# Attention and gated layer on one core: softmax normalised after the product with the values, and nested loops replaced by one straight schedule of slots

## The reference, cut to what matters

```python
# attention: B, H, S, D = 4, 8, 576, 64
scores = scale * np.matmul(q, k.transpose(0, 1, 3, 2))
cum = np.cumsum(np.maximum(s, 0.0), axis=-1)
bias = -(cum[:, :, :, None] - cum[:, :, None, :])
scores = np.where(causal, -1e9, scores + np.minimum(bias, 0.0))
attn = np.exp(scores - scores.max(axis=-1, keepdims=True))
attn = attn / (attn.sum(axis=-1, keepdims=True) + 1e-09)
x = np.matmul(attn, v)                       # heads put side by side: 576 x 512
# gated layer, x_prev is x shifted by one token
k = np.maximum((mu_k * x + (1 - mu_k) * x_prev) @ w_k, 0.0)      # 512 -> 1024
v = k * k @ w_v                                                  # 1024 -> 512
r = 1.0 / (1.0 + np.exp(-((mu_r * x + (1 - mu_r) * x_prev) @ w_r)))
x = r * v
# mixer
u = x + (np.maximum(x.transpose(0, 2, 1) @ w_tok1, 0.0) @ w_tok2).transpose(0, 2, 1)
out = u + np.maximum(u @ w_ch1, 0.0) @ w_ch2
```

## Time and profile before

| | us |
|---|---|
| median of 3 runs | 1021.73 |
| lowest and highest | 1020.29, 1023.51 |
| profiled execution, its span | 1019.8 |
| two turns of attention alone (5.84 to 133.10) | 127.3 |
| six turns of attention beside gated steps (133.10 to 557.80) | 424.7 |
| the last two gated steps and the mixer | 462.0 |
| PE, DVE, ACT, POOL busy over the span | 915.7, 610.7, 387.0, 379.8 |

### The profile page before, as it was taken

How to read it: one execution, slowest core, us unless ns; L and a number is a source line. 1 busy time by engine, 2 the same in 40 slices (tenths; PEclk the granted TensorE clock), 3 DMA queues, 4 the chain that set the end, 5 groups by cost and what they waited for, 6 DMA issues and landing times.

```text
span 1019.8 us, 21589 instructions
## 1 busy us (share of the span) xinstructions
PE 915.7 (90%) x6645; PEld 843.9 (83%) x6645; DVE 610.7 (60%) x1532; ACT 387.0 (38%) x1048; POOL 379.8 (37%) x713
## 2 busy tenths in 40 slices
PE   6777689888889988898888999899999999999997
PEld 4565578777878877787778998899999999999997
DVE  4878867978788788779787764422333142313222
ACT  3555545455455365464563443221112111211110
POOL 4643466576575665655674651800000000000000
PEclk9978779999999899999999999999999999999999
DMA  7412021121121121220201313210001001000000
GB/s 264 123 36 67 17 60 48 31 75 46 46 58 41 41 58 41 66 55 29 64 0 55 128 36 108 87 47 25 1 23 54 15 23 46 23 0 24 1 24 24
DMA packets 79948, 51.19 MB, mean 50 GB/s; under 512 B 60320, under 2 KB 69088, under 8 KB 79904
## 3 DMA queue, kind: packets, MB, share of 16 engines
q1 hardware_dynamic: 79904, 50.63, 16.8%
HBM read 41.10 MB, written 9.51 MB: 50 GB/s over the span
## 4 chain that ended last, share of the span: by engine, by line
PE 60%; DVE 18%; issue 11%; ACT 5%; POOL 3%; DVEq 1%; DMA 1%; SPq 1%; POOLq 0%; ACTq 0%
PE psum L137 48%; PE psum L686 5%; DVE z L1071 3%; ACT z L871 3%; DVE z L1086 3%; PE psum L669 3%; DVE p_t L1094 2%; PE psum L656 2%; DVE z_sum L1080 2%; DVE x_mix L1131 1%; PE psum L789 1%; DVE x_all L1104 1%; PE psum L769 1%; POOL xm_lo L558 1%; DVE z_inv L1082 1%
## 5 line engine op out<-in xcount | busy, mean ns | idle before, releaser
L871 ACT ACTIVATE z<-z,z_min 128x128 f32<-128x128 f32 (+4 forms) x160 | 95.6, 598 | 124.2 <-DVE z_min L1071 124.2
L1230 DVE SCALAR_TENSOR_TENSOR hid_lo<-psum,hid_hi 128x288 fp32r<-128x288 f32 x96 | 43.9, 457 | 131.7 <-ACT hid_hi L989 131.7
L137 PE MATMUL psum<-u_hi,c_hi 128*128 128x288 f32 x384 | 116.1, 302 | 2.9 <-DVE u_lo L1220 2.9
L669 PE MATMUL psum<-ident,z 128*128 128x128 f32 (+2 forms) x480 | 67.1, 276 | 54.5 <-DVE p_t L1094 41.7
L137 PE MATMUL psum<-hid_hi,c_hi 128*128 128x288 f32 x384 | 113.9, 297 | 0.0
L137 PE MATMUL psum<-hid_hi,c_lo 128*128 128x288 f32 x384 | 113.3, 295 | 0.0
L137 PE MATMUL psum<-hid_lo,c_hi 128*128 128x288 f32 x384 | 113.1, 295 | 0.0
L137 PE MATMUL psum<-u_hi,c_lo 128*128 128x288 f32 x384 | 113.1, 295 | 0.0
L137 PE MATMUL psum<-u_lo,c_hi 128*128 128x288 f32 x384 | 113.0, 294 | 0.0
L669 PEld LDWEIGHTS psum<-ident,z 128*128 128x128 f32 (+2 forms) x480 | 48.9, 147 | 76.3 <-issue 76.1
L521 POOL TENSOR_SCALAR z<-cum_k,cum_qp 128x128 f32<-128x128 f32 (+4 forms) x160 | 95.1, 603 | 42.1 <-PE psum L669 22.7
(11 more groups left out here) (114 smaller groups left out, 2462.3 us busy)
## 6 DMA issues: line engine op xcount, KB each, us to landing
cum_k<-cum_scratch SPq DMA_DIRECT2D x32, 288.0 KB, 3.4
q_raw<-in_q SPq DMA_DIRECT2D x32, 144.0 KB, 2.4
k_raw<-in_k SPq DMA_DIRECT2D x32, 144.0 KB, 2.6
mixed_scratch<-gate SPq DMA_DIRECT2D x32, 144.0 KB, 1.8
x_t<-mixed_scratch SPq DMA_DIRECT2D x8, 576.0 KB, 4.4
out<-o_sb SPq DMA_DIRECT2D x24, 192.0 KB, 2.1
v_raw<-in_v SPq DMA_DIRECT2D x32, 128.0 KB, 2.3
c_raw<-in_moe_w_ch SPq DMA_DIRECT2D x4, 768.0 KB, 6.5
```

Of the source, the lines that this page charges most:

```text
L137: done = nc.tensor.matmul(out, w[a][0:r, tw, w_cols], x[b][0:r, tx, x_cols], start=first and n == 0 and m == 0, stop=last and n == len(til ...
L669: done = nc.tensor.transpose(t_bank[h][0:rows(kb), kb * r:(kb + 1) * r], z_view(h, i, kb * P, rows(kb)), ident[0:r, 0:r])
L871: nc.scalar.activation(w, w, ACT.Exp, bias=z_min[0:r, h, i:i + 1], scale=-1.0, accum_out=z_sum[0:r, i, h:h + 1]).then_inc(exp_done[h], 1)
L1230: nc.vector.scalar_tensor_tensor(hid[1][:, f % 3, :], s_bank[f % 2][:, 0:HALF], 0.0, hid[0][:, f % 3, :].bitcast(F32), ALU.max, ALU.subtra ...
```

## The change

It has three parts.

1. **Normalising.** `normalise` goes. The weights are transposed as the exponential left them. DVE computes the reciprocals of the sums per part (`invert`, two small instructions for three or two blocks), POOL copies each reciprocal 64 times side by side (`spread`, into `inv_rep`), PE transposes that into a `t_bank` (`inverses_t`, uses `nA` for part 0 in bank 0 and `nB` for part 1 in bank 1), and `outputs` multiplies the finished `x_all` by it, with one DVE instruction that frees the bank.
2. **Fewer, wider instructions.** One ACT and one DVE instruction splits what one bank holds, often of both heads (`HOLDS`); the first two query blocks are scored in one piece; POOL masks both heads at once; the key block of 64 is padded with zeros (`p_last`).
3. **The schedule.** `TURN` and the loops go. Slots are counted from 0 to 198; `PAIR_AT` says in which slot a pair begins, and the tables `PE_AT`, `ACT_AT`, `DVE_AT`, `POOL_AT` say in which slot after that each engine does which piece. The first four pairs begin every 7 slots and so overlap by four; the gated layer begins in slot 31 instead of 42. After that a turn still has 21 slots and two pairs: one, here called A, begins in slot 18 of the turn before, and the other, B, in slot 7. All waits are for constants. The mixing for a step stands in slots 10 to 20 of the turn before it; two of its eight parts used to stand at the start of the step's own turn. The order in a slot is still: attention, gated layer, mixing.

```diff
-TURN = [[("q", 0, 0)], [("k", 0, 0)], [("s", 0, 0)], [("s", 0, 1)],
...
+GATE_AT = 31
+PERIOD = 7
+PAIR_AT = [PERIOD * p if p < 4 else GATE_AT - 3 + (p - 4) // 2 * TURN_SLOTS + p % 2 * 10 for p in range(PAIRS)]
...
+PE_AT = {0: ["q"], 1: ["k"], 2: ["s1"], 3: ["s2"], 4: ["s3"], 5: ["s4", "w1"], 6: ["s5", "w2"], 7: ["nA", "vA"],
+         8: ["w3"], 9: ["w4"], 10: ["nB", "vB"]}
+ACT_AT = {0: ["q"], 1: ["k"], 2: ["e1"], 3: ["e2"], 4: ["e3"], 5: ["w1"], 6: ["w2", "e5"],
+          8: ["oA", "w3"], 9: ["w4"], 11: ["oB"]}
+DVE_AT = {0: ["q"], 1: ["k"], 2: ["s1"], 3: ["s2"], 4: ["s3"], 5: ["s4", "w1"], 6: ["s5", "w2", "rA"],
+          8: ["oA", "w3"], 9: ["w4", "rB"], 11: ["oB"]}
...
+PE_RANK, ACT_RANK, DVE_RANK, POOL_RANK = "sqkwnv", "oqkwe", "osqkwr", "xbv"
...
+T_USES = {"q": [("q0", 0), ("q1", 1)], "k": [("k0", 0), ("k1", 1)], "w1": [("w0", 0), ("w1", 1)],
+          "w2": [("w2a", 0), ("w2b", 1)], "nA": [("nA", 0)], "w3": [("w3a", 1), ("w3b", 0)],
+          "w4": [("w4a", 1), ("w4b", 0)], "nB": [("nB", 1)]}
...
+            def spread(p, part):
...
+                nc.gpsimd.tensor_copy(inv_rep[:, 0:b - a, :, :],
+                                      z_inv[:, a:b, :].unsqueeze(3).to_broadcast([P, b - a, 2, D])).then_inc(inv_spread, 1)
...
+            def bank_free(p, name):
+
+                if T_NTH[p, name] > 1:
+                    pe.wait_ge(t_free[T_BANK[name]], T_NTH[p, name] - 1)
...
+            def inverses_t(p, part):
+                name = "nA" if part == 0 else "nB"
+                pe.wait_ge(inv_spread, p * 2 + part + 1)
+                bank_free(p, name)
...
-            def normalise(p, i):
...
-                    w = z_view(h, i, 0, n)
-                    nc.vector.tensor_scalar(w, w, z_inv[0:r, i, h:h + 1], None, ALU.mult).then_inc(p_ready[h], 1)
...
+            def outputs(p, part):
...
+                x = x_all[:, x_part(p, part)]
+                nc.vector.tensor_tensor(x, x, t_bank[bank][:, 0:PART_W[part]], ALU.mult).then_inc(t_free[bank], 1)
...
-            with act.Fori(2, STEPS) as j:
-                for u, slot in enumerate(TURN):
-                    for piece, x, i in slot:
-                        attend(j, x, piece, i)
-                    last_mixes(j - 2, u)
-                    gated_turn(j - 2, u, True)
+            for slot in range(TWO_LEFT):
+                attend(slot)
+                if slot in SPLIT_SLOTS:
+                    weight_hi(SPLIT_SLOTS.index(slot))
+                if slot >= GATE_AT:
+                    step, u = divmod(slot - GATE_AT, TURN_SLOTS)
+                    gated(step, u)
+                    mixes(step + 1, u, MIX_IN_TURN)
+                mixes(0, slot, FIRST_MIX)
```

More of the change, by code:

```diff
@@ L36 @@
 EPS = 1e-9
-QA, QB = 3 * P, S - 3 * P
+AT = [min(i * P, S) for i in range(NBLK + 1)]
+SIZE = [AT[i + 1] - AT[i] for i in range(NBLK)]
+Z_AT = [sum(AT[1:i + 1]) for i in range(NBLK + 1)]
+Z_COLS = Z_AT[NBLK]
+PARTS = [(0, 3), (3, NBLK)]
+PART_AT = [AT[a] for a, _ in PARTS]
+PART_W = [AT[b] - AT[a] for a, b in PARTS]
 GROUPS = CT + FT + CT
@@ L77 @@
 LAST_RECIPROCALS = {3 + n: 1 for n in range(2 * CT)}
-MIX = VALUE
 POOL_LO = 3
[L80 to L90, removed]
+GATE_AT = 31
+PERIOD = 7
+PAIR_AT = [PERIOD * p if p < 4 else GATE_AT - 3 + (p - 4) // 2 * TURN_SLOTS + p % 2 * 10 for p in range(PAIRS)]
+LAST_SLOT = GATE_AT + STEPS * TURN_SLOTS
+TWO_LEFT = GATE_AT + (STEPS - 2) * TURN_SLOTS
+FIRST_MIX = [10, 11, 17, 18, 24, 25, 30, 31]
@@ new lines, with count_t_uses @@
+T_BANK = {name: bank for uses in T_USES.values() for name, bank in uses}
+HOLDS = {"w0": (0, (0, 1), 0, 1), "w1": (1, (0, 1), 0, 2), "w2a": (2, (0,), 0, 3), "w2b": (2, (1,), 0, 3),
+         "w3a": (3, (0,), 0, 4), "w3b": (3, (1,), 0, 4), "w4a": (4, (0, 1), 0, 4), "w4b": (4, (0, 1), 4, 5)}
+def count_t_uses():
+    nth, nth_split, seen, split = {}, {}, [0, 0], [0, 0]
+    for slot in range(LAST_SLOT):
+        for p, piece in pieces(PE_AT, PE_RANK, slot):
+            for name, bank in T_USES.get(piece, []):
+                seen[bank] += 1
+                nth[p, name] = seen[bank]
+                if name[0] != "n":
+                    split[bank] += 1
+                    nth_split[p, name] = split[bank]
+    return nth, nth_split, seen
@@ new lines, in weights_t @@
+            def weights_t(p, name):
+                bank = T_BANK[name]
+                i, heads, first, end = HOLDS[name]
+                for h in heads:
+                    pe.wait_ge(exp_done[h], p * NBLK + i + 1)
+                bank_free(p, name)
+                pe.sem_inc(passed["pe"], 1)
+                r = SIZE[i]
+                for n, (h, k) in enumerate((h, k) for h in heads for k in range(first, end)):
+                    keys = z_view(h, i)[:, AT[k]:AT[k + 1]]
+                    done = nc.tensor.transpose(t_bank[bank][0:SIZE[k], n * r:(n + 1) * r], keys, ident[0:r, 0:r])
+                done.then_inc(t_filled[bank], 1)
@@ new lines, in values @@
+            def values(p, part):
+                q_end = PART_AT[part] + PART_W[part]
+                for h in range(2):
+                    if part == 0 and h == 0:
+                        pe.wait_ge(v_split, p + 1)
+                    for name in (("w2a", "w2b"), ("w4a", "w4b"))[part]:
+                        pe.wait_ge(t_free[T_BANK[name]], T_NTH[p, name])
+                    if p or part:
+                        pe.wait_ge(o_added[h], p * 2 + part)
+                    blocks = [b for b in range(NBLK) if AT[b] < q_end]
+                    for b in blocks:
+                        q0 = max(PART_AT[part], AT[b]) - PART_AT[part]
@@ L1183, in last_mixes, with mixes @@
[L1183 to L1193 removed]
+            def mixes(step, slot, at):
+                for m in range(2 * CT):
+                    if at[m] == slot:
+                        mix(step, m)
```

705 lines of the change are left out of this document (337 added, 368 removed), and 5 rows, old and new, of the table TURN.

## The result

The changed kernel takes 1072.02 us (median of 4 runs, 1066.31 to 1078.32), the kernel before in the same session 1022.62: 1.048 times as long, with a 95% interval of 1.0434 to 1.0527. The forecast was 1035, with a range to 1054. The direction was right and the size was not.

A forecast was written before the change was run, and what follows sets the result against it. It took a turn to be bound by PE's own work plus bank hand-overs among PE, ACT and DVE. 1019.8 - 12 + 27 - 2 = 1033 for the span, 1035 for the median; 8-in-10 range 992 to 1054.

The forecast's parts named there:

- part one: Up to the start of the gated layer: gate begins at 121 and not 133.1, -12 us.
- six turns: Turns of attention beside gated steps: more PE idle time and added transposes, +4.5 us a turn, +27 us.
- the rest: After the six turns: step 7's mixing no longer waits at the turn's start, -2 us; otherwise the same.
- median over the profiled span: The median of the runs lies 1.9 us over the profiled span.
- The waits found in the orders: PE's idle time in a turn, read from the order of each engine: 13.1 us against 9.0.
- the period of 27: Part one, slot 10 to slot 31: three periods of 7 slots, one pair each, taken as 27 us each.
- comes and goes: Low clock in part one, given 2 us in the sum for the gate's start.
- The wait for the mixing: Step 7, at the turn's start: the mixing is no longer waited for, -2 us.
- DVE's relief: DVE's busy time: loses some 97 us, and must fall by 90 to 105 in any case.
- The port and the clock: Rival: POOL holds up small DVE instructions, or low clock in each turn, +8 us a turn; 1059 us, chance 0.09.
- The waits go: Rival: waits go with the normalising, new ones mostly covered; -16 us in the turns, -16 in part one; 988, chance 0.27.
- what DVE does as a sum decides nothing by itself: In a turn: the limit is PE's own work plus moments when PE, ACT and DVE hand a bank around.

The follow-up runs named there:

- e10: Changed kernel with 7, 4 and 7 transposes for nobody ahead of three waits of PE in a turn; 1038.1 us.
- e6: Kernel before the change with its normalising product cut to one column, weights left unnormalised; 977.5 us.
- e2: Changed kernel with 14, 8 and 14 transposes for nobody ahead of three waits of PE in a turn; 1035.5 us.
- e11: Kernel before the change with one more DVE instruction a pair, ahead of the normalising, to lengthen a wait of PE; 1043.7 us.
- e7: Changed kernel with 12 instead of 4 transposes for nobody at the end of each slot of part one; 1060.6 us.
- e3: Changed kernel without its normalising: no reciprocals, copies, transposes or products of them, outputs left unnormalised; 950.5 us.
- e9: Changed kernel's order and wider instructions with the old normalising of the weights on DVE ahead of the transposes; 1020.2 us.
- e5: Changed kernel with ACT's copy of the output's lo half one slot earlier and PE's values ahead of the reciprocals' transposes; 983.7 us.
- e1: Changed kernel with only ACT's copy of the output's lo half one slot earlier, ahead of that slot's gated reads; 1036.1 us.
- e12: Changed kernel with 14 transposes for nobody ahead of the third weights' second half alone; 1066.2 us.

## Why the prediction was wrong, step by step

| term | forecast | measured |
|---|---|---|
| part one | -12 | +2.8 |
| six turns | +27 | +38.7 |
| the rest | -2 | +3.1 |
| median over the profiled span | 1.9 | 7.6 |

The last line is no term of the kernel: the profiled execution, at 1066.3, was the shortest of the four runs. The four differences, 14.8, 11.7, 5.1 and 5.7, make up the 37 us between 1035 and 1072.

- **The waits found in the orders: right.** 13.1 us of idle time a turn were listed, and 10.8 were measured; 4.5 was taken as net with the transposes. At the full clock a turn grew from 68.4 to 72.0 (e10), by 3.6, or 21.5 in six turns. The orders of four engines, with durations from the trace, gave each of the five large waits to 0.6 us; of the small ones about half came (0.45 for 0.9, 0.50 for 1.0). One small slip: at 1.07 us for eight, five transposes are 0.67 us and not 0.55, 0.2 more a turn.
- **The step that failed is the clock, which the sum took as unchanged.** "Such a reading counts some waits that swallow one another, so I take +4.5", with the low clock only at the end of the range and in a rival at 0.09. Measured: the six turns stood 28.9 us over six times 71.97, where before it was 11.6 over six times 68.39. The 17 between them are the clock; with the 21.5 that is the 38.7. This split is an estimate: in e6, at the full clock, every second turn of the old order takes 1.3 more (64.6 for 63.3), and with that the clock's part is 21 and the rest 18. The hint was there: the list held two waits of 2.4, longer than any in the earlier trace rows, and the prediction itself set a turn at 0.93 beside one at 1.00. e2 and e10 show that filling the waits gives the clock back, and e11 that longer ones cost it in the old kernel.
- **Part one: 15 us off.** The gate began at 136.8, outside the 108 to 134 given for it; the same code began it between 133.6 and 140.3, so some 3 of the 15 can be chance. Slot 10 began at 42.5 and not at 38, as pair 0's values and the keys' bank come in between: 4.5. From there to the gate it took 94.3 and not 83. In e7, at a clock of 0.97, the same stretch took 85.4, so 9 of the 11 are the clock again, as far as two single profiles show, and the period of 27 was nearly right (28.5). That the low clock "comes and goes" for 2 us was the mis-sized term.
- **The rest: 5 us off.** The wait for the mixing, 1.7 us, went as forecast. But PE waited 1.49 us for a read of the gate in step 6, and 2.02 for a `k_lo` on DVE where it had been 0.46. No run tries this; that they come from what else DVE and ACT do at those places is argued.
- **DVE's relief: 72 and not 97 us**, outside the 90 to 105 given "in any case". The new instructions cost as forecast (product 0.543 and 0.35, POOL's copy 0.6) or less (the small ones 11.0 us in all for 16), each form for itself:

```profile
L571 POOL COPY inv_rep<-z_inv 128x384 f32<-128x384 f32 x16 | 8.8, 551 | 49.1 <-DVE z_inv L1109 49.1
```

```profile
L1129 DVE TENSOR_TENSOR x_all<-x_all,psum 128x384 f32<-128x384 f32 x16 | 8.9, 555 | 2.2
L1129 DVE TENSOR_TENSOR x_all<-x_all,psum 128x192 f32<-128x192 f32 x16 | 5.7, 355 | 2.5 <-DVE x_all L1121 0.5
...
L1107 DVE TENSOR_SCALAR z_sum<-z_sum 128x4 f32<-128x4 f32 x16 | 2.7, 166 | 0.0
```

  But others grew. The two lines are the same mix, before and after:

```profile
L1131 DVE SCALAR_TENSOR_TENSOR x_mix<-x_all,mu,x_mix 128x288 f32<-128x288 f32 x64 | 38.3, 610 | 2.5 <-POOL x_mix L551 1.9
```

```profile
L1160 DVE SCALAR_TENSOR_TENSOR x_mix<-x_all,mu,x_mix 128x288 f32<-128x288 f32 x64 | 51.8, 812 | 14.1 <-POOL x_mix L595 14.1
```

  With 64 of these (13.5 us), 40 `k_lo` (0.525 to 0.652, 5.1) and 32 sums for the gate (0.361 to 0.477, 3.7) that is 22 us, most of what is missing. All three read and write SBUF, beside POOL's work, which the new order has put elsewhere. It isn't POOL's new copies: in e3 and e9, which have the new order without them, the same mix took 0.759 and 0.718 us. The Trainium skill, "SBUF — State Buffer" (SBUF: two separate sides), says that DVE with two SBUF inputs and a GpSimd instruction that reads SBUF shut each other out for a whole instruction; the first two have two such inputs and fit it, the gate's sum has one. No run here tries it alone.
- **The rivals.** "The port and the clock" named 0.92 as its point; the clock was 0.91, so its second half came true, at 1072 for its 1059. Its first half did not: the small instructions in front of the reciprocals became shorter, 0.343 to 0.16, not longer. "The waits go" failed as placed. e5, with the pieces placed elsewhere, takes 983.7, near its 988, but that is partly luck: its turns gave 33.6 us against that rival's 16, its part one 9.3 against 16, and the rest grew by 3. And "what DVE does as a sum decides nothing by itself" is contradicted for the old order by e6, where work taken off DVE gave 44 us.
- **Not tried.** No run keeps the loops or the narrow instructions in the new order, so what these two parts of the change gave by themselves is not shown. The rule of the Trainium skill, "Runtime: NRT & Kernel Launch" (Instruction fetch mechanics), that the prediction cites is for a taken branch whose target lies outside the current two-page window of instructions, a condition that the prediction left out.

## What to carry to other kernels

Sum up idle time, but list the single waits of PE by length too: waits that grow, the longest from 1.7 to 2.5 us, can cost nearly three times their own growth, most of it in half-speed matmuls behind them (e11: 17.0 us for 6.2). Before an operation is moved into a shared bank, ask who frees that bank and what stands ahead of the freeing instruction on an in-order engine; here one slot and a later place in it on ACT, and one swap on PE, were worth 88 us. And where PE has to wait, work for nobody in that place is a quick test of whether the clock is what is being paid.

## What was not expected of the hardware

- Seven, four and seven transposes in front of three waits were enough to keep the clock at 2.4 GHz for a whole turn (e10, 1.00 for 0.89). The Trainium skill, "TensorE: Matmul & The Clock Gate" (Part 4: PE-mode transpose), says that transposes don't count as busy in the way matmuls do; these runs disagree, as do the 12 transposes a slot of e7 (0.97 for 0.76). Before them, though, stood matmuls in both.
- The clock fell behind single waits of 2.46 (e11) and 2.49 us, and behind ones of 1.81 (e1) and 1.30 (after). It did not fall behind waits of 2.48 (e11) and 2.34 (e12), nor behind 1.78 and 1.83 (e10). A longer wait makes the fall likelier, and no wait of up to 2.5 us made it certain; behind the six waits of 3.7 to 4.2 us in e9 it fell each time.
